# Squared rows of x taken back from HBM and turned 32 by 32 on VectorE, in place of TensorE's transposes, in five of six blocks

## The reference

```python
def _attn_ref(q, k, v):                       # 2 batches, 8 heads, 768 tokens, head size 64
    k_sum = k.reshape(B, H, nb, block, D).max(axis=3)
    v_sum = v.reshape(B, H, nb, block, D).mean(axis=3)
    ...
    return np.matmul(a, v_all)                # softmax over a window of 31 keys and 24 summaries

def _moe_ref(x, w_in, w_out):                 # x 1536x512, w_in 512x2048, w_out 2048x512
    h = x @ w_in
    g = np.where(h > 0.0, h, alpha * (np.exp(np.minimum(h, 0.0)) - 1.0))
    return g @ w_out

def _moe2_ref(x, expert_emb, tau, w1, w2):    # 8 experts, w1 8x512x1024, w2 8x1024x512
    xn = x / (np.linalg.norm(x, axis=-1, keepdims=True) + 1e-06)
    en = expert_emb / (np.linalg.norm(expert_emb, axis=-1, keepdims=True) + 1e-06)
    logits = xn @ en.T / tau
    expert_idx = np.argmax(logits, axis=1)
    ...
        h = np.maximum(x[mask] @ w1[e], 0.0)
        out[mask] = gate_w[mask, None] * (h @ w2[e])
```

## Time and profile before

| | |
|---|---|
| median of three runs | 536.41 us (536.21 to 536.44) |
| span of the profiled execution | 534.9 us |
| TensorE (PE) busy | 522.5 us, 98% |
| VectorE (DVE) busy | 311.8 us, 58% |
| ScalarE (ACT) busy | 225.5 us, 42% |
| GpSimd (POOL) busy | 91.5 us, 17% |
| mean granted TensorE clock | 0.996 of full speed |

### The profile page before, as it was taken

The page is one execution under the profiler, slowest core; times in us unless marked ns, Lnnn a source line. Parts: engine busy times, 40 slices in busy tenths (PEclk is TensorE's granted clock), DMA queues, the critical chain, the costliest instruction groups (busy, mean ns, idle before and its releaser), DMA issues.

```text
span 534.9 us, 11689 instructions
## 1 busy us (share of the span) xinstructions
PE 522.5 (98%) x3858; PEld 450.1 (84%) x3859; DVE 311.8 (58%) x691; ACT 225.5 (42%) x506; POOL 91.5 (17%) x221
## 2 busy tenths in 40 slices
PE   8799999999999999999999999999999999999995
PEld 7688888888888888888888899888788888888883
DVE  3779898557754565457543567768492374222662
ACT  5677764443543343334432545451351352111440
POOL 6413140032210000000000000101312221111221
PEclk9999999999999999999999999999999999999998
DMA  8999220444211112111000900010955155101000
GB/s 210 266 334 315 47 49 12 94 84 98 78 41 25 22 23 63 25 21 54 3 1 1 354 0 2 22 60 10 364 206 198 44 199 188 39 28 36 20 20 25
DMA packets 78220, 49.24 MB, mean 92 GB/s; under 512 B 61014, under 2 KB 66134, under 8 KB 78176
## 3 DMA queue, kind: packets, MB, share of 16 engines
q1 hardware_dynamic: 75776, 42.37, 27.1%
q0 software_dynamic: 2400, 6.30, 3.6%
HBM read 43.40 MB, written 6.82 MB: 94 GB/s over the span
## 4 chain that ended last, share of the span: by engine, by line
PE 95%; ACT 1%; issue 1%; DMA 1%; SPq 0%; DVE 0%; POOLq 0%; DVEq 0%; ACTq 0%
PE bank L1010 25%; PE bank L1054 9%; PE bank L1061 8%; PE bank L1067 8%; PE bank L1219 5%; PE bank L1265 5%; PE bank L1227 5%; PE bank L1273 5%; PE bank L1221 5%; PE bank L1267 5%; PE bank L988 3%; PE bank L970 3%; PE bank L961 2%; PE bank L1257 2%; PE bank L1120 1%; PE bank L1075 1%
## 5 line engine op out<-in xcount | busy, mean ns | idle before, releaser
L1420 ACT ACTIVATE el<-bank 128x512 f32<-128x512 f32 x48 | 28.6, 596 | 112.5 <-PE bank L1010 112.2
L1738 DVE TENSOR_SCALAR el<-el 128x512 f32<-128x512 f32 x48 | 21.1, 440 | 74.7 <-ACT el L1420 74.7
L1010 PE MATMUL bank<-x_hi,w_hi_parts 128*128 128x256 f32 x376 | 61.1, 285 | 0.0
L1010 PE MATMUL bank<-x_hi,w_lo_parts 128*128 128x256 f32 x376 | 60.2, 282 | 0.0
L1010 PE MATMUL bank<-x_lo,w_hi_parts 128*128 128x256 f32 x376 | 60.1, 282 | 0.0
L1010 PEld LDWEIGHTS bank<-x_hi,w_hi_parts 128*128 128x128 f32 x376 | 53.5, 188 | 3.8 <-issue 0.2
L1054 PE MATMUL bank<-w_hi_parts,g_hi 128*128 128x512 f32 x192 | 54.9, 407 | 0.0
L1061 PE MATMUL bank<-w_lo_parts,g_hi 128*128 128x512 f32 x192 | 52.6, 396 | 0.0
L1067 PE MATMUL bank<-w_hi_parts,g_lo 128*128 128x512 f32 x192 | 52.3, 394 | 0.0
L752 POOL COPY kb<-kT 128x96 f32<-128x96 f32 x96 | 26.2, 315 | 148.3 <-PE bank L961 127.9
L1010 PEld LDWEIGHTS bank<-x_lo,w_hi_parts 128*128 128x128 f32 x376 | 51.4, 188 | 0.0
(11 more groups left out here) (288 smaller groups left out, 905.7 us busy)
## 6 DMA issues: line engine op xcount, KB each, us to landing
raw<-in_moe_w SPq DMA_DIRECT2D x8, 2048.0 KB, 7.6
w_raw<-in_moe_w_in SPq DMA_DIRECT2D x8, 512.0 KB, 6.0
w_raw<-in_moe_w_out SPq DMA_DIRECT2D x8, 512.0 KB, 6.6
v_raw<-in_v SPq DMA_DIRECT2D x8, 384.0 KB, 4.0
x_rows<-x SPq DMA_DIRECT2D x6, 512.0 KB, 3.1
vwin<-in_v SPq DMA_DIRECT2D x32, 72.0 KB, 2.1
q_raw<-in_q SPq DMA_DIRECT2D x64, 32.0 KB, 1.9
k_raw<-in_k SPq DMA_DIRECT2D x8, 192.0 KB, 3.2
```

Source lines behind the costliest of these rows:

```text
L1010: mm = pe.matmul(o, r32(w[:, at:at + P]), r32(x[i % 2][:, c, :]), start=(part == "hh" and c == 0), stop=(part == "lh" and c == DC - 1))
L1420: act.activation(el[n % 2], bank[:, H_BANK[n % 2], :], ACT.Exp).then_inc(e_act, 1)
```

## The change

The rows of x that a block has just written to HBM are read back into `x2` itself, in pieces of 32 rows, so that they lie there as squares of 32 by 32; VectorE turns all squares in one instruction into `x2T`. TensorE's `route_turn` and ScalarE's `store_x2T` remain for block 5 alone. `squares` goes from place +12 to +2, since it must read `x2` before it is overwritten. Partition p of chunk c now holds column 4p + c of x and not 128c + p, so that the expert rows and block 5 are read with a step of four elements (`of_chunk`).

```diff
-    def r_at(i, t):
-        return PER_BLOCK * (i + 1) + (9 if (i, t) == (NB - 3, 1) else 3 + 4 * t)
+    def x2_at(i):
+        return PER_BLOCK * (i + 1) + 6
...
     def sq_at(i):
-        return PER_BLOCK * (i + 1) + 12
+        return PER_BLOCK * (i + 1) + 2
...
-    T_TURNS = sorted([(r_at(i, t), 0, i * QT + t) for i in range(NB - 1) for t in range(QT)]
-                     + [(d_at(i), 1, i) for i in range(NB - 1)]
+    T_TURNS = sorted([(d_at(i), 1, i) for i in range(NB - 1)]
...
+        x2_squares = x2.rearrange("p t n -> p (t n)")
...
+        def of_chunk(rows, c):
+
+            return rows.rearrange("p (m k) -> p k m", k=DC)[:, c, :]
...
+            def load_x2(i):
+
+                sp.wait_ge(st_x, 16 * (i + 1))
+                sp.wait_ge(ss_a, QT * (i + 1))
+                for r in range(GROUPS):
+                    sp.dma_start(x2_squares[r * SQ:(r + 1) * SQ, :].rearrange("p (c d) -> p c d", d=P),
+                                 x_rows[i * TB:(i + 1) * TB, r * P:(r + 1) * P].rearrange("(c p) d -> p c d", p=SQ)
+                                 ).then_inc(ld_x2, 16)
...
             store_x2(0)
+            load_x2(0)
             load_k1(1)
...
                     if u == PAIRS * j:
                         store_x2(j - 3)
+                        load_x2(j - 3)
             store_x2(NB - 3)
+            load_x2(NB - 3)
...
             store_x2(NB - 2)
+            load_x2(NB - 2)
             store_x2(NB - 1)
...
-            def route_turn(i, t, b):
-
-                pe.wait_ge((acc_a, acc_d)[t], i + 1)
+            def route_turn(t, b):
+
+                pe.wait_ge((acc_a, acc_d)[t], NB)
                 for c in range(DC):
-                    mm = pe.transpose(bank[:, b, c * P:(c + 1) * P], x2[:, t, c * P:(c + 1) * P], ident[:, :])
+                    mm = pe.transpose(bank[:, b, c * P:(c + 1) * P], of_chunk(x2[:, t, :], c), ident[:, :])
                 mm.then_inc(r_t, 1)
...
             def route_dots(i, b):
-                pe.wait_ge(x2T_ev, QT * (i + 1))
+                if i < NB - 1:
+                    pe.wait_ge(x2_turned, i + 1)
+                else:
+                    pe.wait_ge(x2T_ev, QT)
...
                 for i in range(NB - 1):
-                    for t in range(QT):
-                        if r_at(i, t) == place:
-                            t_bank_free(place, 0)
-                            route_turn(i, t, T_BANK)
                     if d_at(i) == place:
...
             def store_acc(i):
                 act.wait_ge(y_mm, STEPS * (i + 1))
                 if i > 0:
-                    act.wait_ge(st_x, 16 * i)
-                    act.wait_ge(r_t, QT * i)
-                    act.wait_ge(ss_a, QT * i)
+                    act.wait_ge(x2_turned, i)
...
+            def turn_x2(i):
+
+                dve.wait_ge(ld_x2, 16 * GROUPS * (i + 1))
+                if i > 0:
+                    dve.wait_ge(r_mm, i)
+                dve.transpose(x2T.rearrange("p t g c n -> p (t g) c n"),
+                              x2_squares.rearrange("p (t d c) -> p t c d", c=DC, d=GROUP)).then_inc(x2_turned, 1)
...
                 for i in range(NB - 1):
+                    if x2_at(i) == place:
+                        turn_x2(i)
                     if d_at(i) == place:
```

More of the change, by code:

```diff
@@ L255, in zone @@
                         a = scope.enter_context(nc.sbuf_tensor(buf, shape, F32))
-                        out.append(a[:, :] if len(shape) == 2 else a[:, :, :] if len(shape) == 3 else a[:, :, :, :])
+                        out.append(a[:, :] if len(shape) == 2 else a[:, :, :] if len(shape) == 3 else
+                                   a[:, :, :, :] if len(shape) == 4 else a[:, :, :, :, :])
                 sizes.append(sum(int(np.prod(shape[1:])) for shape in group.values()))
@@ L327, in build @@
             {"x_hi1": [P, DC, TB], "x_lo1": [P, DC, TB], "g_hi0": [P, 2 * TB], "g_hi1": [P, 2 * TB],
-             "el0": [P, 2 * TB], "el1": [P, 2 * TB], "x2": [P, QT, DM], "x2T": [P, QT, DC, P]},
+             "el0": [P, 2 * TB], "el1": [P, 2 * TB], "x2": [P, QT, DM], "x2T": [P, QT, GROUPS, DC, GROUP]},
             {"until_el": [P, 2 * DC * TB + 4 * TB], "g_lo0": [P, 2 * TB], "g_lo1": [P, 2 * TB]},
@@ L367, in build @@
             "h_mm e_act e_min g_v g_hi_a g_ev y_mm acc_a acc_d")
-        ss_a, r_t, x2T_ev, r_mm, l_ev = sems(
-            "ss_a r_t x2T_ev r_mm l_ev")
+        ss_a, ld_x2, x2_turned, r_t, x2T_ev, r_mm, l_ev = sems(
+            "ss_a ld_x2 x2_turned r_t x2T_ev r_mm l_ev")
         oh_v, rank_mm, rank_v, root_a, lgd_v, sm_a, gate_v, star_v, list_v, list_mm, list_ok = sems(
@@ L827, in _ @@
             pool.wait_ge(st_x, 16 * NB)
-            pool.wait_ge(r_t, NT)
+            pool.wait_ge(r_t, QT)
             pool.wait_ge(ss_a, NT)
@@ L898, in t_bank_free @@
                     _, kind, n = T_TURNS[at - 1]
-                    pe.wait_ge((x2T_ev, l_ev, pT_ev, rank_v, list_ok, emb_enT)[kind], n + 1)
+                    pe.wait_ge({1: l_ev, 2: pT_ev, 3: rank_v, 4: list_ok, 5: emb_enT}[kind], n + 1)
             def o_bank_free(place, kind):
@@ L1084, in route_dots @@
                         mm = pe.matmul(bank[g * GROUP:g * GROUP + E, b, 0:QT * GROUP], enT[:, c, :],
-                                       x2T[:, :, c, g * GROUP:(g + 1) * GROUP],
-                                       start=(c == 0), stop=(c == DC - 1))
+                                       x2T[:, :, g, c, :], start=(c == 0), stop=(c == DC - 1))
                 mm.then_inc(r_mm, 1)
@@ L1110, in transpose_embeddings @@
                 for c in range(DC):
-                    mm = pe.transpose(bank[:, T_BANK, c * E:(c + 1) * E], emb_n[0:E, c * P:(c + 1) * P],
+                    mm = pe.transpose(bank[:, T_BANK, c * E:(c + 1) * E], of_chunk(emb_n[0:E, :], c),
                                       ident[0:E, 0:E])
@@ L1299, in _ @@
             up_half(0, 0, 0).then_inc(h1_half, 1)
-            route_turn(NB - 1, 0, O_BANK)
-            route_turn(NB - 1, 1, S_BANK[1])
+            route_turn(0, O_BANK)
+            route_turn(1, S_BANK[1])
             transpose_x(1)
@@ L1430, in store_acc, with store_x2T @@
                 if i > 0:
-                    act.wait_ge(st_x, 16 * i)
-                    act.wait_ge(r_t, QT * i)
-                    act.wait_ge(ss_a, QT * i)
+                    act.wait_ge(x2_turned, i)
                 act.copy(x2[:, 0, :], bank[:, ACC[0], :]).then_inc(acc_a, 1)
[L1436 to L1441, removed]
+            def store_x2T(t, b):
+                act.wait_ge(r_t, t + 1)
+                act.wait_ge(r_mm, NB - 1)
+                act.copy(x2T[:, t, :, :, :].rearrange("p g c n -> p c g n"),
+                         bank[:, b, :].rearrange("p (c g n) -> p c g n", c=DC, n=GROUP)).then_inc(x2T_ev, 1)
             def squares(i, t):
@@ L1445, in squares @@
                 if i < NB - 1:
-                    act.wait_ge(r_mm, i + 1)
-                    squared = x2T[:, t, :, :].rearrange("p c n -> p (c n)")
+                    if i > 0:
+                        act.wait_ge(r_mm, i)
+                    else:
+                        act.wait_ge(emb_t, 1)
+                    squared = x2T[:, t, :, :, :].rearrange("p g c n -> p (g c n)")
                 else:
@@ L1472, in behind @@
                     for t in range(QT):
-                        if r_at(i, t) == place:
-                            store_x2T(i, t, T_BANK)
                         if sq_at(i) == place:
@@ L1580, in _ @@
             roots(1)
-            store_x2T(NB - 1, 0, O_BANK)
-            store_x2T(NB - 1, 1, S_BANK[1])
+            store_x2T(0, O_BANK)
+            store_x2T(1, S_BANK[1])
             def relu_halves(s):
@@ L1749, in store_acc @@
                 if i > 0:
-                    dve.wait_ge(st_x, 16 * i)
-                    dve.wait_ge(r_t, QT * i)
-                    dve.wait_ge(ss_a, QT * i)
+                    dve.wait_ge(x2_turned, i)
                 dve.tensor_copy(x2[:, 1, :], bank[:, ACC[1], :]).then_inc(acc_d, 1)
+            def turn_x2(i):
+                dve.wait_ge(ld_x2, 16 * GROUPS * (i + 1))
+                if i > 0:
+                    dve.wait_ge(r_mm, i)
+                dve.transpose(x2T.rearrange("p t g c n -> p (t g) c n"),
+                              x2_squares.rearrange("p (t d c) -> p t c d", c=DC, d=GROUP)).then_inc(x2_turned, 1)
             def store_dots(i, b):
```

## The result

The changed kernel took 533.04 us (median of 4 runs, 532.35 to 533.52) beside 536.31 us before (536.12 to 536.44): a ratio of 0.9932, 95% interval 0.9916 to 0.9947. The profiled execution took 532.35 us by itself, with a span of 530.5 us.

What follows compares the result with a forecast made beforehand. The prediction took TensorE, busy 522.5 of 534.9 us, as the bound. Ten transpose groups gone save 4.2 us, all else costs 0: 536.41 - 4.2 = 532.2 us, range 531.2 to 533.7.

Steps and rivals of the forecast that it cites:

- What bounds the kernel: In the 48 steps TensorE is always busy; no other engine ends a wait of it, so removed TensorE work saves time.
- Ten groups, 4.2 us: TensorE loses ten groups of four transposes: seven beside attention units at 0.38 us, three without at 0.48; taken as 4.2 us.
- rival of 5.8 us of busy time: TensorE's 40 removed transposes save their full busy time, 5.8 us, giving 530.6 us; chance 0.05.
- ScalarE, nothing: Ten copies go and ten squares move to +2, hidden in idle time of at least 3.19 us: no cost.
- VectorE, nothing at 1.24 us: Each new turn takes 1.24 us, at most 4.4; block 4, the tightest, has room for 4.8 us: no cost.
- SP's queue, nothing: Loads behind `load_x2` wait with it, but keys and queries still land about 2 us before VectorE turns them: no cost.
- three places: SP's queue in block 0 (keys, 2 us of room), block 2 (queries, 2.2 us), and blocks 3 and 4 (nothing soon needed).
- slower rival: SP's queue becomes the bound in blocks 0 to 2, holding up keys and queries: some 538 us; chance 0.05.
- Strided reads: Twelve transposes' weight loads take twice 140 ns, adding 1.7 us behind the last step: 533.9 us; chance 0.10; forecast took no cost.
- signs of being wrong: TensorE waiting for VectorE or ScalarE within the steps, or steps' length changing where nothing was taken out.
- The sum: ScalarE, VectorE and SP's queue 0 each, TensorE's groups minus 4.2 us: 536.41 - 4.2 = 532.2 us.

Runs made afterwards that it cites:

- idle_turns: The changed kernel with four never-read transposes of the identity put back on TensorE at each of the ten places: 536.90 us, ratio 1.0007 to the kernel before.
- turn_four: The changed kernel with VectorE's turn done four times over in each block: 540.09 us, ratio 1.0068 to the kernel before.
- short_pieces: The changed kernel with each piece of x loaded by 16 DMAs of 128-byte runs instead of 4 of 512, all reads dense: 532.71 us, ratio 0.9927.
- late_squares: The changed kernel with the squares at place +4 and VectorE's turn at +8, one step later each: 532.63 us, ratio 0.9940 to the kernel before.
- again: The changed kernel run once more without edit, beside the kernel before: 532.29 us, ratio 0.9925.
- look_b: The changed kernel executed once more without edit, to catch a long execution in the profile: 533.88 us.

## Why the prediction was right

I had put 532.2 us, and a range of 531.2 to 533.7; 533.04 us was measured first, and the eleven executions of this kernel in all lie between 531.99 and 533.88, with a median of 532.36; one of them, the longest, lies above the range.

- **What bounds the kernel.** Right. TensorE has no idle time in the steps of either kernel, and `idle_turns`, which gives back TensorE's groups alone, gives back the whole time.
- **Ten groups, 4.2 us.** The mechanism was right, the term 0.2 to 0.3 us too small: 4.44 us by the steps, 4.51 by `idle_turns`. What mis-sized it was the choice of neighbours. These are the two pairs of the earlier trace rows and the second pair of the earlier trace rows in the changed kernel, each from `hidden` to `hidden`:

```profile
139.83 0.64 PE L1029 MATMUL bank<-x_hi,w_hi_parts 128*128 128x256 f32 x4
...
147.29 0.64 PE L1029 MATMUL bank<-x_hi,w_hi_parts 128*128 128x256 f32 x4
...
153.44 0.63 PE L1029 MATMUL bank<-x_hi,w_hi_parts 128*128 128x256 f32 x4
...
160.84 0.63 PE L1029 MATMUL bank<-x_hi,w_hi_parts 128*128 128x256 f32 x4
```

```profile
310.32 0.64 PE L1029 MATMUL bank<-x_hi,w_hi_parts 128*128 128x256 f32 x4
...
315.99 0.64 PE L1029 MATMUL bank<-x_hi,w_hi_parts 128*128 128x256 f32 x4
```

Without a turn the two steps of the earlier trace rows are 7.46 and 7.40 us long, so they were never alike, and the group in the second cost 7.83 - 7.40 = 0.43 us, not 0.38. The step of the earlier trace rows is 5.67 us, and its group cost 0.45, not 0.48. Nor do groups without attention units beside them cost more, as I had argued: taken so, the seven beside units cost 0.40 to 0.49 us, 0.44 on average, and the other three 0.40, 0.45 and 0.46, 0.44 on average too. The rival of 5.8 us of busy time is out.
- **ScalarE, nothing.** Right: the squares ran from 96.86 to 98.2 us and 2.75 us of idle time were left behind them, and `idle_turns` shows that its missing copies gave nothing.
- **VectorE, nothing at 1.24 us.** The cost was right, the duration was not: 2.07 us, inside the bounds of 1.24 and 4.4. `turn_four` shows the room I had counted for it in block 4, 4.8 us, to 0.1 us.
- **SP's queue, nothing.** Right for the change as made. The account of the three places was incomplete: the tightest path behind a hold is neither keys nor queries but the v rows that GpSimd adds up, at a room of 3.8 us from the end of the sum to TensorE; `short_pieces` and `late_squares` found it. The slower rival would have needed much more than that.
- **Strided reads.** I took nothing and gave them a tenth for 1.7 us. They were real: 0.24 us for the expert rows (a step of 6.41 us in place of 6.17), some 0.07 us for block 5's eight, which hide most of their loads (0.95 us from start to the next kind in place of 0.88). Together 0.3 us, so the case lay between my forecast and the rival. The rival put all twelve transposes behind the last step, but the four of the expert rows stand within the 48 steps, at 94.4 us. With them one of my signs of being wrong came true: a step's length changed where nothing was taken out. I had given it no term in the sum. The Trainium skill, "SBUF — State Buffer", in its note on cachelines, has accesses that each cross to a new 16-byte line pay a penalty; this case agrees, with 2.07 against 1.24 us on VectorE and 0.211 against 0.140 us for a load of weights. Only steps of one and of four elements were run, so that it is the crossing of lines of 16 bytes isn't shown.
- **The sum.** 4.44 - 0.24 - 0.07 = 4.1 us, so two errors of about the same size, the group's price and the strided reads, cancelled, and that the 4.2 us came out so closely is luck; the spans of the two profiled executions differ by 0.2 to 0.3 us more, which is no more than starts differ by between executions. The first median lay at 533.04, 0.8 us above the number, because two of its four executions were long ones (up to 533.52); on the chip of `again` the medians differ by 536.53 - 532.29 = 4.24 us. The long ones weren't profiled; in the long one that was, `look_b`, most of it is the start.

## What to carry to other kernels

Where one engine is busy all the time, price what is taken from it by the same step in a stream, with and without the instructions, never by their busy time, and take several pairs, since neighbours differ: two steps with the same kinds of work were 0.06 us apart, a seventh of what was to be measured. Work moved to another engine or queue is free up to the room behind it; count that room to the first instruction of the bound engine that would wait, and along every path behind a queue that is held, not only the nearest. When executions of one kernel fall in two groups, cut the span at landmarks before tying the gap to the change.

## What the runs showed of the hardware

- VectorE's 32x32 turn of 128x1024 fp32 took 1.24 us with dense reads and 2.07 us with a step of four elements within a block: 1.04 and 1.86 ns a column beside 0.17 us fixed (from the shorter turns of the earlier trace rows; for the strided one the same fixed part is assumed).
- Loads of weights of 128x128 fp32 took 0.140 us dense and 0.211 us with a step of four, those of 8 rows 0.136 and 0.213. With eight of 128 rows in a row only 0.07 us of the 0.57 us more showed in TensorE's stream, with four of 8 rows 0.24 of 0.31 us. Why the short ones lost more wasn't tried.
- Four fp32 transposes cost TensorE's stream 0.40 to 0.49 us, 0.44 to 0.45 on average, while the profile shows 0.272 us for each of them.
- After a wait of 3.45 us (`turn_four`) TensorE worked at a granted clock of 0.50, the level of 1.2 GHz, from 337.31 to 339.18 us and of 0.64 on average from there to 340.56, which cost 1.4 us beside the wait itself. After waits of 0.2 and 0.8 us (`late_squares`, `short_pieces`) the next steps were as long as ever.
